# Which engine's queue starts the loads of v in a fused attention and mixture-of-experts kernel

## The reference

```
scores = q @ k.T / sqrt(64)
keep   = is_sink | (0 <= rel < 128)
a      = softmax(where(keep, scores, -1e9))
x      = a @ v                     # heads side by side: 1536 tokens x 512
```

## Time and profile before

| What | Value |
|---|---|
| Three runs, us | 1378.34, 1374.97, 1379.07 (median 1378.34) |
| The profiled execution, us | 1376.82, with a span of 1375.0 |
| Mean granted TensorE clock | 0.991 of full speed |
| PE busy | 1335.9 us, 97% |
| DVE, ACT, POOL busy | 500.2, 261.5, 319.8 us |
| DMA queues | q1 55.28 MB, q10 1.39 MB |

### The profile page before, as it was taken

The page is one execution under the profiler, slowest core; times in us unless marked ns, Lnnn a source line. Parts: engine busy times, 40 slices in busy tenths (PEclk is TensorE's granted clock), DMA queues, the critical chain, the costliest instruction groups (busy, mean ns, idle before and its releaser), DMA issues.

```text
span 1375.0 us, 16253 instructions
## 1 busy us (share of the span) xinstructions
PE 1335.9 (97%) x6103; PEld 1091.8 (79%) x6103; DVE 500.2 (36%) x964; ACT 261.5 (19%) x555; POOL 319.8 (23%) x179
## 2 busy tenths in 40 slices
PE   5888999998999999999999999999999999999999
PEld 5656678876888888888888888888888888888887
DVE  6888553435522222323222222222222223232322
ACT  5655543421110101010202010101011010101020
POOL 6555021133011111111222221111111111111110
PEclk9988999999999999999999999999999999999999
DMA  5443100001000000000000001100000000000002
GB/s 166 145 140 99 64 0 1 1 31 61 0 31 31 31 31 31 31 31 31 31 31 31 31 32 41 48 31 31 31 31 31 31 31 31 31 31 31 31 0 92
DMA packets 15988, 56.94 MB, mean 41 GB/s; under 512 B 2144, under 2 KB 4192, under 8 KB 11872
## 3 DMA queue, kind: packets, MB, share of 16 engines
q1 hardware_dynamic: 14848, 55.28, 11.5%
q10 hardware_dynamic: 1120, 1.39, 0.3%
HBM read 53.51 MB, written 3.15 MB: 41 GB/s over the span
## 4 chain that ended last, share of the span: by engine, by line
PE 91%; DVE 5%; issue 2%; ACT 1%; DMA 0%; DVEq 0%; ACTq 0%; SPq 0%
PE ps L493 28%; PE ps L495 28%; PE ps L494 28%; PE ps L473 2%; DVE probs L931 2%; PE ps L436 2%; PE ps L407 1%; PE ps L578 1%; DVE probs L908 1%; PE ps L408 1%; PE ps L482 1%; DVE acc L1040 0%; ACT acc L814 0%; PE ps L412 0%; DVE gate L1130 0%
## 5 line engine op out<-in xcount | busy, mean ns | idle before, releaser
L493 PE MATMUL ps<-w_unit,h_hi 128*128 128x512 f32 x768 | 298.9, 389 | 0.0
L495 PE MATMUL ps<-w_unit,h_lo 128*128 128x512 f32 x768 | 298.8, 389 | 0.0
L494 PE MATMUL ps<-w_unit,h_hi 128*128 128x512 f32 x768 | 298.8, 389 | 0.0
L886 ACT ACTIVATE h_hi<-ps 128x512 fp32r<-128x512 f32 x192 | 114.9, 598 | 908.7 <-PE ps L495 908.7
L493 PE MATMUL ps<-x_hi,w_unit 128*128 128x512 f32 x720 | 280.1, 389 | 0.0
L494 PE MATMUL ps<-x_lo,w_unit 128*128 128x512 f32 x720 | 280.1, 389 | 0.0
L495 PE MATMUL ps<-x_hi,w_unit 128*128 128x512 f32 x720 | 280.1, 389 | 0.0
L1184 DVE SCALAR_TENSOR_TENSOR acc<-ps,gate_now,acc 128x512 f32<-128x512 f32 x192 | 144.2, 751 | 355.5 <-PE ps L495 355.5
L1109 DVE SCALAR_TENSOR_TENSOR h_lo<-ps,h_hi 128x512 fp32r<-128x512 f32 x192 | 132.8, 692 | 385.5 <-ACT h_hi L886 385.5
L373 POOL TENSOR_SCALAR w_unit<-w_raw 128x2048 fp32r<-128x2048 f32 x31 | 59.5, 1919 | 813.6 <-PE ps L495 808.4
L493 PEld LDWEIGHTS ps<-w_unit,h_hi 128*128 128x128 f32 x768 | 144.1, 188 | 30.0
(11 more groups left out here) (129 smaller groups left out, 1108.6 us busy)
## 6 DMA issues: line engine op xcount, KB each, us to landing
w_raw<-w_exp SPq DMA_DIRECT2D x32, 1024.0 KB, 4.8
q_raw<-qT SPq DMA_DIRECT2D x16, 384.0 KB, 4.3
k_raw<-kT SPq DMA_DIRECT2D x16, 384.0 KB, 4.0
out<-acc SPq DMA_DIRECT2D x12, 256.0 KB, 2.0
w_raw<-w_in SPq DMA_DIRECT2D x8, 256.0 KB, 2.7
w_raw<-w_out SPq DMA_DIRECT2D x8, 256.0 KB, 2.9
v_sb<-v SPq DMA_DIRECT2D x9, 192.0 KB, 3.6
v_sb<-v ACTq DMA_DIRECT2D x7, 192.0 KB, 2.4
```

Source lines behind the costliest of these rows:

```text
L493: pe.matmul(o, ws[0], xs[0], start=first, stop=False)
L494: pe.matmul(o, ws[0], xs[1], start=False, stop=False)
L495: return pe.matmul(o, ws[1], xs[0], start=False, stop=last)
L886: act.activation(h_hi[:, g, :], bank(g % 4), ACT.Relu).then_inc(h_hi_out, 1)
```

## The change

The loads that ScalarE started behind `round_x` are started by SyncE, at the end of `load_beside`, behind a wait for `x_full`. ScalarE's two helpers and their calls go. Sizes, destinations, semaphores of the loads and their order among themselves stay.

```
                 load_segments(i)
                 sp.wait_ge(va_used, i)
                 sp.dma_start(v_sb[:, 0, :], v[i, 0]).then_inc(v_loaded[0], 16)
+                sp.wait_ge(x_full, i)
+                sp.dma_start(v_sb[:, 1, :], v[i, 1]).then_inc(v_loaded[1], 16)
+                for h in range(2):
+                    sp.dma_start(v_sink[h * NS:(h + 1) * NS, h * DH:(h + 1) * DH],
+                                 v[i, h, 0:NS, 0:DH]).then_inc(vs_loaded, 16)
...
-            def load_v(p, h):
-                act.dma_start(v_sb[:, h, :], v[p, h]).then_inc(v_loaded[h], 16)
-
-            def load_sinks(p):
-                for h in range(2):
-                    act.dma_start(v_sink[h * NS:(h + 1) * NS, h * DH:(h + 1) * DH],
-                                  v[p, h, 0:NS, 0:DH]).then_inc(vs_loaded, 16)
...
                     if k == 2 and before:
                         round_x(i - 1)
-                        load_v(i, 1)
-                        load_sinks(i)
...
             round_x(last_pair - 1)
-            load_v(last_pair, 1)
-            load_sinks(last_pair)
```

## The result

The changed kernel takes 1390.88 us in the median of nine runs (1384.62 to 1393.45), against 1378.34 before, the median of nine as well (1374.97 to 1385.89). The ratio of the two is 1.0089 with a 95% interval of 1.0068 to 1.0109, that is 12.3 us slower (9.4 to 15.0). The forecast was 1384.5 with a range of 1376.7 to 1391.4 and slower as the likeliest outcome. The direction was right and half of the size was missing. The profiled execution took 1384.62 us, with a span of 1382.8, and was the fastest of the nine.

What follows compares the result with a forecast made beforehand. TensorE's chain bounds the kernel, with VectorE setting the attention stage's pace from step 4; five bodies at 1.24 us gave +6.2, so 1378.3 + 6.2 = 1384.5 us, range 1376.7 to 1391.4.

Steps and rivals of the forecast that it cites:

- ScalarE's relief: ScalarE loses three DMA issues, 0.27 us ahead of an exponential; gain hidden, counted 0, at most -1.6 us.
- When q lands: In body(2), q issued about 64.25, landing 3.0 us later at 67.3, late end 68.3; GpSimd's split 1.9 to 2.9 late.
- The replay: VectorE's body(2) retraced with GpSimd starting at 67.3: shifted stops behind GpSimd's instructions make the next body 1.24 us late.
- a landing at 68.3: Late end for q in body(2): GpSimd's second head follows at once, over three more VectorE instructions, about +2.6 us.
- the cited rule: Trainium skill: VectorE instruction with two SBUF inputs contends with GpSimd reading SBUF; the second to issue waits for the whole first.
- L945 would be blocked: VectorE's L945, 0.68 us with GpSimd idle, was counted as stopping behind GpSimd, like L923.
- The step: Counting of bodies: 4 or 5 times 1.24, 5.0 to 6.2 us; TensorE's new gap near a fallen clock decided for +6.2.
- rival 4: Added idling drops the clock in more bodies, 1.6 to 3.0 us each; 1391.4 us and above; chance 0.06.
- 1: Attention-stage loads are late but cost nothing, as GpSimd idles 2.82 us between heads; 1378.3 us; chance 0.22.
- 3: L945 and L950 do not stop, so step 8 keeps its place; 1378.3 us; chance counted within rival 1's 0.22.
- 2: Faster by ScalarE: exponentials of steps 3 to 5 come 0.27 us earlier; 1376.7 or 1373.7 us; chance 0.12.

Runs made afterwards that it cites:

- second profile: The changed kernel unedited, measured and profiled again: 1390.29 us, ratio 1.0085 to the kernel before.
- the first experiment: The changed kernel, but SyncE starts the next pair's q and k loads ahead of the wait for x_full and the moved loads: 1378.6 us, ratio 1.0010.
- the wait alone: The kernel before, but SyncE waits for x_full instead of va_used ahead of the first head's v; ScalarE's loads stay: 1384.76 us, ratio 1.0058.
- GpSimd later: The kernel before, loads untouched, but GpSimd's first split of a body waits for the scores of step 6 instead of step 5: 1395.33 us, ratio 1.0144.

## Why the prediction was right, and what it missed

- **ScalarE's relief is hidden.** Right: with the order of loads restored the kernel is as before (1.0010).
- **When q lands.** Right: issue at `pv_sinks` + 1.8, landing 3.1 later, GpSimd at + 5.06 (forecast 4.8, up to 5.8). The split stays in time for TensorE.
- **The replay.** Right in kind, wrong in its path. Right: L916 stands 1.5 us, TensorE gets no wait for a split, and the loss vanishes with short GpSimd instructions (1350.8 against 1351.5). Wrong: it had L945 behind GpSimd's `k_lo`, with step 8's `mask_max` 1.52 us late by it and GpSimd's second head 1.24 late. L945 slipped in ahead and held GpSimd up. Step 8's `mask_max` was not late, and GpSimd's second head, 11.2 to 11.6 us behind `pv_sinks` at full clock, was where it had been (11.4), now with 0.17 us of idling or none before it. The lateness came behind that, in the `normalise` of step 8 and, where GpSimd did not idle, in L950 and the `normalise` of step 9. That the second head follows at once was forecast only for a landing at 68.3, at +2.6 us. Measured at full clock are 0.5, 1.3 and 1.4 us a body. That 1.24 lies among them is luck.
- **Which instructions the cited rule covers.** The prediction counted L931 with L923 as agreeing with the rule for two SBUF inputs. L931 reads one tensor and a column of factors, so it is no case of that rule; that it stands all the same is what the rows show.
- **L945 would be blocked.** Right, shown with two pieces (1.49 us). In the changed kernel it came first, and its twin L950 was blocked (1.30 us). The Trainium skill, SBUF — State Buffer, "Who interferes with whom", has both sides of it: whoever issues first gets the shared ports for the whole instruction. The trace agrees, with GpSimd's 2.34 us instead of 1.80.
- **The clock: the term that was mis-sized.** The step said that more idling would speak for the fallen clock and took it as the reason to count five bodies instead of four, 1.2 us. The rest was rival 4, at 0.06 and 1.6 to 3.0 us for a fall. Measured, the loss is 12.3 us, and five bodies at 0.5 to 1.4 are 2.5 to 7. The replay's own figures had a hint: it showed a gap of 1 us opening in step 11, and I did not ask what it adds up to ahead of the next `turn`. The idle time there went from 2.2 us to between 3.6 and 4.0 in one body of the first profile and four of the second, and in all five the clock fell. Four of these bodies last 21.3 to 22.9 us, 1.5 to 3 more than 19.8. The fifth is body 6, which the prediction left out because it has no split: the fall cost 6.4 us there.
- **Rivals.** 1 and 3 (late but free) are refuted by the result, and so is 2's time; 2's mechanism leaves no trace in the first experiment. Rival 4's mechanism was at work beside the forecast's, not instead of it. I had made the two exclusive.
- **The range.** The median lies 0.5 us inside its upper end, which was set where rival 4 begins. With that rival's mechanism at work, this is luck.

How much of the 12.3 us is stops and how much the clock is not settled for the median, since no kernel here holds the clock. In the second profile at least 6.4 of 13.3 us are the clock's (body 6). A comparison at one mean granted clock over the span doesn't settle it: at 0.983, four runs of the changed kernel took 1387.9 to 1393.1 us and three of the kernel before 1383.2 to 1383.9, some 6 us apart; at 0.985 it was 1384.6 against 1381.3 and 1383.4.

## What to carry to other kernels

A wait put into a queue's program delays every transfer that is started behind it, so moving a load is priced by what it is now in front of. Here the load itself was free, and putting it behind q and k cost nothing that could be measured. An idle stretch of TensorE is priced by what comes behind it, too: one that grew from 2.2 to 4.0 us was followed by 6.4 us lost to the low clock in a body that was otherwise unchanged. When VectorE and GpSimd work on SBUF at the same time, look at durations, not at waits: an instruction of 16 columns that takes 174 to 1647 ns is standing behind the other engine, and the place and length of the other's instructions are costs even if that engine idles. Cutting GpSimd's 768-column instructions in two gained more (1.2%) than the studied change lost.

## What was not expected of the hardware

- GpSimd's cost of a cut: one rounding of 128x768 takes 0.83 us in one instruction, 1.02 in two, 1.15 in three and 1.62 in six, so some 0.16 us for each instruction more. It sets how fine a cut pays.
- The stops go both ways: GpSimd's 1.80 us `k_lo` took 2.34 us behind VectorE's L938.
- How sharply TensorE's granted clock went with the idle time ahead of a body: after 3.6 to 4.0 us it fell to half in all five cases of the two profiles of the changed kernel, and in all seven with the wait alone and with GpSimd later; after 2.2 to 2.7 us, in the kernel before and the first profile after, it fell in three of six, and in one of two with the wait alone. In body 1 of the first profile it fell inside the body, behind 1.41 us.
- Landing time of 384 KB depended on how close a transfer ran ahead of it: for q of the first head, 2.9 to 3.1 us in the ten bodies of the changed kernel's two profiles, with v (192 KB) started 1.6 us earlier, and 3.3 to 3.9 in the five with the wait alone, with v started 0.88 us earlier.
